# First units normalised and turned with shorter lags, biases one at a time, step 2's weight parts behind step 1, and the last two units' values together

## The reference

```
q, k, v: (2 batches, 8 heads, 768 positions, 64)
scores = q k^T / 8 - slope[head] * distance, kept for key < 8 or 0 <= query - key < 96
a = softmax(scores);  x = a v, laid out as (1536, 512)
h = x w_in1;  x = (h * sigmoid(h)) w_out1          # (512, 2048), (2048, 512)
h = x w_in2;  out = (h * clip(h + 3, 0, 6) / 6) w_out2
```

## Time and profile before

| | |
|---|---|
| median of 3 runs | 608.09 us (607.88 to 610.44) |
| profiled execution | 607.72 us, span 606.0 us |
| TensorE busy | 594.7 us, 98% |
| VectorE, ScalarE, GpSimd busy | 369.2, 341.6, 284.1 us |
| DMA | 50.05 MB, mean 83 GB/s |

### The profile page before, as it was taken

How to read it: one execution, slowest core, us unless ns; L and a number is a source line. 1 busy time by engine, 2 the same in 40 slices (tenths; PEclk the granted TensorE clock), 3 DMA queues, 4 the chain that set the end, 5 groups by cost and what they waited for, 6 DMA issues and landing times.

```text
span 606.0 us, 9614 instructions
## 1 busy us (share of the span) xinstructions
PE 594.7 (98%) x3429; PEld 516.4 (85%) x3429; DVE 369.2 (61%) x696; ACT 341.6 (56%) x659; POOL 284.1 (47%) x353
## 2 busy tenths in 40 slices
PE   8999999799999999999999999999999999999998
PEld 5665568799999999999999998888888988898896
DVE  6678886655755568557555865575557685554331
ACT  6889885544454466444444675545447565555441
POOL 4787995656933314439433144394333343331110
PEclk9999999899999999999999999999999999999999
DMA  8435330032222113221211123212221252221002
GB/s 351 162 110 206 110 117 5 34 138 70 71 70 70 70 35 105 70 69 37 88 59 64 38 70 101 71 36 104 70 69 36 70 175 70 69 70 35 1 1 104
DMA packets 14595, 50.05 MB, mean 83 GB/s; under 512 B 1618, under 2 KB 1874, under 8 KB 14546
## 3 DMA queue, kind: packets, MB, share of 16 engines
q1 hardware_dynamic: 14258, 48.63, 23.4%
q10 hardware_dynamic: 288, 0.79, 0.4%
HBM read 46.27 MB, written 3.15 MB: 82 GB/s over the span
## 4 chain that ended last, share of the span: by engine, by line
PE 88%; POOL 6%; ACT 2%; DVE 2%; issue 1%; DMA 0%; DVEq 0%; ACTq 0%
PE ps L954 38%; PE ps L1031 22%; PE ps L1022 14%; PE ps L1023 8%; POOL probs L291 3%; PE ps L926 2%; PE ps L911 2%; PE ps L901 2%; POOL rsume L283 1%; ACT probs L680 1%; POOL wo_lo L336 0%; POOL x_t L323 0%; POOL x_t L328 0%; DVE x_lo L472 0%; DVE g_f L488 0%
## 5 line engine op out<-in xcount | busy, mean ns | idle before, releaser
L336 POOL TENSOR_TENSOR wo_lo<-wo_raw,wo_hi 128x1024 fp32r<-128x1024 f32 x32 | 76.6, 2395 | 265.7 <-ACT wo_hi L748 258.3
L954 PE MATMUL ps<-x_hi,wi_hi 128*128 128x384 f32 x448 | 151.6, 338 | 4.1 <-ACT u_c L728 3.1
L954 PE MATMUL ps<-x_hi,wi_lo 128*128 128x384 f32 x448 | 150.6, 336 | 0.0
L954 PE MATMUL ps<-x_lo,wi_hi 128*128 128x384 f32 x448 | 150.4, 336 | 0.0
L478 DVE TENSOR_TENSOR c_sb<-ps,p_c 128x384 f32<-128x384 f32 x64 | 35.6, 557 | 166.4 <-PE ps L954 166.1
L728 ACT ACTIVATE p_c<-ps 128x384 f32<-128x384 f32 x64 | 31.5, 492 | 132.3 <-PE ps L954 132.1
L954 PEld LDWEIGHTS ps<-x_hi,wi_hi 128*128 128x128 f32 x448 | 84.6, 189 | 8.0 <-ACT u_c L728 4.3
L954 PEld LDWEIGHTS ps<-x_hi,wi_lo 128*128 128x128 f32 x448 | 84.5, 189 | 0.7
L954 PEld LDWEIGHTS ps<-x_lo,wi_hi 128*128 128x128 f32 x448 | 84.5, 189 | 0.0
L1031 PE MATMUL ps<-wo_hi,g_lo 128*128 128x512 f32 (+1 forms) x194 | 76.3, 393 | 0.0
L1031 PE MATMUL ps<-wo_lo,g_hi 128*128 128x512 f32 (+1 forms) x194 | 76.3, 393 | 0.0
(11 more groups left out here) (94 smaller groups left out, 1091.0 us busy)
## 6 DMA issues: line engine op xcount, KB each, us to landing
wi_raw<-in_w_in SPq DMA_DIRECT2D x32, 512.0 KB, 3.3
wo_raw<-in_w_out SPq DMA_DIRECT2D x32, 512.0 KB, 3.4
v_raw<-in_v SPq DMA_DIRECT2D x8, 704.0 KB, 4.2
k_raw<-in_kT SPq DMA_DIRECT2D x8, 464.0 KB, 5.0
out_y<-y_out SPq DMA_DIRECT2D x11, 256.0 KB, 4.4
q_raw<-in_qT SPq DMA_DIRECT2D x6, 384.0 KB, 5.5
q_raw<-in_qT ACTq DMA_DIRECT2D x2, 384.0 KB, 4.0
out_y<-y_out SPq DMA_DIRECT2D x2, 128.0 KB, 1.9
```

The costliest lines, as they stand in the source:

```text
L336: nc.gpsimd.tensor_tensor(wo_lo[:, s % 2, :], wo_raw[:, s % 2, :], wo_hi[:, s % 2, :], ALU.subtract).then_inc(wo_lo_ok, 1)
L954: mm = nc.tensor.matmul(p_bank(bank), w[:, s % 2, at], x[:, b, k, :], start=fresh and k == 0 and i == 0, stop=k == 1 and i == 2, skip_grou ...
```

## The change

Four edits of order; no operation is added or taken away.

- In the first units the lags are shorter. `norm(u)` for u = 0 to 4 follows `total(u)` in the same round, 5 and 6 come one round later, and from round 9 the lag is 2 as before. `turn_probs` of 0 to 4 stand in rounds 3, 4, 5, 7 and 8, with the values of the unit before behind each, and from round 10 the lag is 5 as before. VectorE's `inverse(0)` and `inverse(1)` stand behind negated(1, 1) and negated(2, 1).
- The biases of the next iteration are made one in each of two rounds (u = 3 and 4, 9 and 10, 15 and 16).
- `w_high(2, 0)` and `w_low(2, 0)` go behind step 1's g_high and g_low, next to part 1.
- `values(46)` moves behind P4 of step 0, in front of `values(47)`.

```diff
--- before.py
+++ after.py
@@ -29,6 +29,9 @@
 LAG = 5
 DEEP = 7
 
+SOON_NORM = {0: 0, 1: 1, 2: 2, 3: 3, 4: 4, 6: 5, 7: 6}
+SOON_TURN = {3: 0, 4: 1, 5: 2, 7: 3, 8: 4}
+
 X_SUMS = (30, 33, 35, 38, 41, 44)
 X_HIGHS = (32, 35, 40, 42, 44)
 X_LOWS = (34, 37, 41, 43, 46)
@@ -54,6 +57,16 @@
 LAST = ((0, 0, slice(0, DM)), (1, 1, slice(0, DM)), (2, 2, slice(0, DM)), (3, 3, slice(0, DM)),
         (4, 4, slice(0, QC)), (5, 5, slice(0, DM)), (6, 4, slice(QC, DM)))
 LAST_DVE = (1, 3, 6)
+
+
+def normed(u):
+
+    return SOON_NORM.get(u) if u < 9 else u - 2
+
+
+def turned(u):
+
+    return SOON_TURN.get(u) if u < 10 else u - LAG
 
 
 def at_least(eng, sem, value):
@@ -354,8 +367,8 @@
             def banded():
                 for u in range(NU):
                     total(u)
-                    if u >= 2:
-                        norm(u - 2)
+                    if normed(u) is not None:
+                        norm(normed(u))
                     if 8 <= u < 24 and u % 2:
                         w_sum((u - 8) // 8, (u - 8) // 2 % 4)
                     if u in X_SUMS:
@@ -516,13 +529,15 @@
                     if u % NT == 0 and 0 < u < 4 * NT:
                         dve.wait_ge(bias_ok, 2 * (u // NT) + 1)
                     negated(u, 0)
-                    if u >= 2:
+                    if u >= 4:
                         inverse(u - 2)
                     if u == 0:
                         dve.wait_ge(bias_ok, 1)
                     negated(u, 1)
-                    if u >= LAG and (u - LAG) % 3:
-                        copy_t(u - LAG)
+                    if u in (1, 2):
+                        inverse(u - 1)
+                    if turned(u) is not None and turned(u) % 3:
+                        copy_t(turned(u))
                     if 20 <= u < 36 and u % 4 == 0:
                         w_low((u - 20) // 8, (u - 20) // 4 % 2)
                     if u in X_LOWS:
@@ -635,7 +650,6 @@
                 c_sum(s, 0, 1, p1_c, P2)
                 if s == 1:
                     g_low(0, 1)
-                    w_low(2, 0)
                 if evict:
                     w_low(s + 1, 1)
                     y_copy(blk - 1, 5)
@@ -649,6 +663,7 @@
                 g_low(s, 0)
                 g_low(s, 1)
                 if s == 1:
+                    w_low(2, 0)
                     w_low(2, 1)
                 if f == STEPS - 1 and s < NSTEP - 1:
                     for i in range(7):
@@ -681,11 +696,10 @@
                                          bias=negmax[:, u % DEEP, h:h + 1], scale=-1.0,
                                          accum_out=rsum[:, u % DEEP, h:h + 1]).then_inc(exp_done, 1)
 
-            def bias(it):
-
-                for h in range(0 if it else 1, 2):
-                    nc.scalar.activation(m_bias[:, 2 * it + h, :], m_base[:, :], ACT.Copy,
-                                         scale=slope[:, 2 * it + h:2 * it + h + 1]).then_inc(bias_ok, 1)
+            def bias(it, h):
+
+                nc.scalar.activation(m_bias[:, 2 * it + h, :], m_base[:, :], ACT.Copy,
+                                     scale=slope[:, 2 * it + h:2 * it + h + 1]).then_inc(bias_ok, 1)
 
             def copy_t(u):
                 act.wait_ge(pt_done, u + 1)
@@ -749,13 +763,13 @@
 
             def banded():
                 act.wait_ge(base_ok, 1)
-                bias(0)
+                bias(0, 1)
                 for u in range(NU):
-                    if u >= LAG and (u - LAG) % 3 == 0:
-                        copy_t(u - LAG)
+                    if turned(u) is not None and turned(u) % 3 == 0:
+                        copy_t(turned(u))
                     exps(u)
-                    if u % NT == 1 and u < 3 * NT:
-                        bias(u // NT + 1)
+                    if u % NT in (3, 4) and u < 3 * NT:
+                        bias(u // NT + 1, u % NT - 3)
                     if u % 3 == 2 and u >= 8:
                         x_copy(u // 3 - 2)
                     if 18 <= u < 34 and u % 4 == 2:
@@ -842,8 +856,6 @@
                 blk, f = s // STEPS, s % STEPS
                 evict = blk > 0 and f == 1
                 keep(s, p1_c, 0, P1)
-                if s == 1:
-                    w_high(2, 0)
                 if evict:
                     w_high(s + 1, 1)
                     y_copy(blk - 1, 2)
@@ -858,6 +870,7 @@
                 g_high(s, 0)
                 g_high(s, 1)
                 if s == 1:
+                    w_high(2, 0)
                     w_high(2, 1)
                 if f == STEPS - 1 and s < NSTEP - 1:
                     for i in range(7):
@@ -959,10 +972,10 @@
             def banded():
                 for u in range(NU):
                     scores(u)
-                    if u >= LAG:
-                        turn_probs(u - LAG)
-                    if u >= LAG + 1:
-                        values(u - LAG - 1)
+                    if turned(u) is not None:
+                        turn_probs(turned(u))
+                        if turned(u):
+                            values(turned(u) - 1)
                 values(NU - 6)
                 turn_probs(NU - 5)
                 pe.wait_ge(neg_done, 2 * NU)
@@ -975,9 +988,10 @@
                 turn_probs(NU - 2)
                 values(NU - 3)
                 turn_probs(NU - 1)
-                values(NU - 2)
                 for n in range(P6, P4 + 1):
                     product(0, n)
+
+                values(NU - 2)
                 values(NU - 1)
 
             def general():
```

## The result

The changed kernel took 600.93 us at the median of four runs (600.91 to 601.74). The kernel before, run beside it, took 607.99 (607.88 to 610.44). The two medians are 7.06 us apart, a ratio of 0.9884; the estimate of the ratio on record is 0.9872, with a 95% interval of [0.9846, 0.9898], so the change made the kernel faster by 1.3%, give or take 0.3%. The forecast of 602.1 us stood for 1.0%. The profiled execution took 600.91 us around a span of 599.2, that is 6.81 us less than the profiled one of before, where I had reckoned 6.0.

A forecast was written before the change was run, and what follows sets the result against it. Outside the start and the hand-over from attention to feed-forward, TensorE's pace was taken to bound the kernel. Start 1.3 plus hand-over 4.7 gave 6.0 us off the 608.09 median: 602.1 us, range 600.6 to 604.4.

The forecast's parts named there:

- The cause of the hole: Hand-over: keep(1, u2_c), queued behind ScalarE's w_high(2, 0) that waited for GpSimd, delays P7; TensorE idle 3.05 us.
- The walk of the start: First units: instruction-by-instruction times of the new order, putting scores(10) at 18.8 us instead of 19.98.
- The start: First units: earlier norms and turns bring scores(10) forward by 1.3 us, bounds 0 and 2.0; 1.6 at TensorE's full rate.
- The pair: Values(46) and (47) together behind step 0's P4: silu and wo_low(0) come earlier, P5 of step 1 0.57 us earlier.
- The wait in front of step 2: P1 of step 2 waits 0.6 us for VectorE's w_low(2), delayed by meeting GpSimd; hand-over gain 4.7 instead of 5.27 us.
- The clock: Step 1's P7 to P4: the clock that fell in the idle time returns, 1.5 us of the 4.67 there.
- A: Start: round trips take what the earlier norm gives, so no gain there; 603.4 us; 22% together with B.
- B: Start: TensorE stays slow longer, waiting in small pieces; start worth -0.2 us, time 603.6; 22% together with A.
- C: Step 2: GpSimd and VectorE don't meet; 601.5 us; 19% together with a better start.
- D: Hand-over: w_low(2) 3 us later than reckoned eats the gain; 605.1 us, or 606.6 if the clock falls; 6%.
- E: Hand-over: w_low(2, 1) ready 6 us later than reckoned makes the kernel slower, about 609.6 us or more; 3%.
- The load of step 4's weights: Behind step 2: waits for w_low(2, 1), arrives about 3.7 us after step 2 begins; costed at nothing, cover 2 to 3 us.

The follow-up runs named there:

- weights: Kernel before with only w_high(2, 0) and w_low(2, 0) moved behind step 1's g_high and g_low: 604.54 us, ratio 0.9916.
- weights_dve: Kernel before with only VectorE's w_low(2, 0) moved behind g_low(1), ScalarE's w_high(2, 0) left in place: 609.04 us, ratio 1.0008.
- filled: Kernel before with 20 transposes of the identity into a free PSUM bank in front of P7 of step 1: 607.48 us, ratio 0.9982.
- part 1: The edit moving w_high(2, 0) and w_low(2, 0) behind step 1's g_high and g_low; alone on the kernel before: 604.54 us.
- no_pair: Changed kernel with values(46) put back in front of step 0's products: 601.92 us, ratio 0.9881.
- quiet: Changed kernel with GpSimd's wo_low(1) held back until six low parts of wi are done: 602.81 us, ratio 0.9893.
- start: Kernel before with only the short lags in the first units and the biases one at a time: 606.27 us, ratio 0.9947.
- warm_before: Kernel before with 8 instead of 5 warm-up transposes just ahead of the first scores: 610.01 us, ratio 1.0009.
- part 2: The edits at the start, short lags in the first units and biases one at a time; alone on the kernel before: 606.27 us.
- values: Kernel before with only values(46) moved behind P4 of step 0: 607.80 us, ratio 0.9982.

## Why the prediction was right and where it was off

**Right.** The places: nothing moved outside the start and the hand-over, and the 482.3 to 482.5 us behind them shifted as a block. The cause of the hole: weights and weights_dve show ScalarE's queue. That its clock comes back with it: filled, by the pace of its matmuls. That wo_low(0) moves ahead with the pair: P5 stayed 3.67 us behind P1 of step 1. That part 1 makes a new wait for wi_lo: it was there in weights, no_pair and the changed kernel, and gone in quiet. Its mechanism, two engines that stop each other, was shown by quiet. The walk of the start was close: turns 0 to 3 forecast at 10.0 or a little before, 10.9, 12.8 and 15.2 stood at 9.40, 10.91, 12.50 and 14.73, and scores(10) at 18.25 where 18.8 was forecast.

**The step that failed** is the last one of the sum, and with it the price of the clock as a constant: "The profiled execution took 607.72 us around its span of 606.0, 0.4 below the median 608.09; I take the difference from the median." The mechanisms held; what was mis-sized is what TensorE's clock costs the kernel before. I put it at 1.5 us behind P7's wait in every execution, and took the rest of the clock as the same in all. The runs showed 1.5 to 2.8 us behind that wait, another 1.2 at the start in one trace, and in a few executions nothing. The first of the terms below is off by the clock as well.

**Off in size, four terms.**

- The start: 1.3 us forecast, 1.81 in the profiled execution. With slow loads it is 1.11 (start), with fast ones 1.81. I took the slow rate of the earlier trace rows as a property of the stretch, and as no matter of the clock because the column shows no fall. It is the lower level ahead of the first clock record. When the full clock comes differs between executions of the same code, and my 1.3 lay between its two cases; that the changed kernel was profiled with an early one, at 4.89 us, was luck. For TensorE at its full rate the prediction had 1.6.
- The pair: 0.57 forecast, 0.77 measured. The 0.18 is the shorter step from a turn into a product.
- The wait in front of step 2: 0.6 forecast, 0.24 measured. I had three silus with GpSimd's sums between them end at 113.1 for a down product at 110.05, 3.05 behind it; they ended at 110.71, 2.57 behind 108.14. The two g_low (3.04) and the first two of the four w_low (2.08 of 4.08) then gave the rest.
- The clock: 1.5 us forecast, 1.48 in the pair of profiles. As a number it held there; as a constant it was wrong. From P7 to the down product the traces of kernels with the old wait left empty have 4.60 to 5.92 us against 3.12, so 1.5 to 2.8 us go to the clock there; in the trace of warm_before 1.2 us more went at the start; and in three runs of 60, at 606.4 to 606.6 us, next to nothing. The kernel after has no such fall in its four runs. Its profile stands for all its runs, while the profile of before stands for its faster ones: 6.8 us by the two profiles, 7.1 by the first medians, and about 8 against the 60 later runs (609.0 to 609.2 less 600.9). A range built on 0.4 us of scatter was too narrow on the low side: the ratio 0.9872 puts 608.09 at 600.3.

The first three make the profiles differ by 0.5 + 0.2 + 0.4 more than forecast, less 0.07 for the first scores and 0.14 behind step 2's start: 0.9 us, against the 0.8 from 6.0 to 6.81. What the ratio gives beyond that, another 1.0 us (608.09 - 600.3 is 7.8), is not in the two profiles. I put it down to the clock's scatter in the runs of before. That is argued from the mean clocks of the later runs and not shown, for the clocks of the first four runs of before are not on record.

**The rivals.** A (the start gives nothing) fell with start, 0.9947 with 1.11 us in the trace. B (a slow rate for longer) fell as a rule: the full clock came at 4.89 to 12.27 us in the traces with the new lags and at 9.38 to 12.61 in those with the old ones, and no trace with part 2 shows a recorded fall at the start; the one that does (warm_before) has the old start. In the one execution of start it did come later than in the profile of before (12.27 against 11.34), and even there 1.11 us were won. C gave a time nearer than the forecast, 601.5, but for a wrong reason: the engines do meet. D and E needed a late w_low(2, 1), and it was 0.24 us late. The load of step 4's weights came 3.72 us behind the start of step 2 (GpSimd's first sum of them at 120.44), as forecast (3.7), and its cover held: the rest of the kernel took as long as before.

**Open.** What decides when in the first 13 us TensorE gets its full clock. The longer warm-up did not (7.30, 9.84 and 9.66 us with it). Where the clock fell in the runs without a trace, and why an idle of 1.06 us brought it down once where 1.00 did not, stay open too. Nor was it tried to place the meeting of wo_low and VectorE somewhere without a price; splitting wo_low would be the next attempt.

## What to carry to other kernels

When an engine waits, look first at what stands ahead of the late instruction in its own in-order queue: here a rounding of weights needed 14 us later held up a copy of half a microsecond for which TensorE stood still. Price a hole as its wait plus the clock that falls behind it, and treat that second part as a distribution and not a number: compare the times and mean clocks of many runs before the profile's difference is laid on a median. Check a clock of 1.00 in a profile by the length of equal instructions; where the trace has no record it stands for nothing. And ask of every moved instruction whom it meets at its new place; the meeting of GpSimd and VectorE only moved when it was pushed.

## What the runs showed of the hardware

- 20 transposes in TensorE's wait (2.35 us of work, 0.88 of idle time left) kept the full pace of the 18 matmuls behind it (3.24 us), where behind an idle of 3.05 us the granted clock was at 0.50 and they took 4.60.
- After an idle of 1.06 us in a thinly used stretch (warm_before) the clock fell as well, and stayed down for more than 3 us; idles of 1.00 and 1.01 us at the same place (values, weights, filled) and of 0.73 us in front of step 1 did not do this.
- In all 13 traces with clock records TensorE started at its lower clock and got the full one at 4.89 to 12.61 us, at times that differ between executions of the same code: weight loads of scores of 282 to 336 ns ahead of it, 182 to 189 behind it. The profile has no clock record ahead of that point and prints 1.00.
- Where VectorE's instructions with two SBUF inputs met GpSimd's, both paid: in quiet one w_low took 3.29 us instead of 1.09 and wo_low 3.18 instead of 2.40.
